# Weight splits and block 0's transposes as steps of each engine's order, with the orders laid out anew, in a two-stage MLP kernel on one core

## The reference

```python
# attention part: a causal depthwise convolution with 7 softmaxed taps per token and head
w = softmax(weight_gen)                     # (2, 4096, 8 heads, 7 taps)
out = einsum('bshk,bskhg->bshg', w, windows of x)   # (2, 4096, 192)
x = out.reshape(8192, 192)
# first MLP
h = x @ w_in                                # 192 -> 2048
P = a[0] + a[1]*h + a[2]*h**2 + a[3]*h**3
Q = 1 + |b[0]|*|h| + |b[1]|*h**2
x = (P / (Q + 1e-6)) @ w_out                # 2048 -> 192
# second MLP
xn = x / rms(x) * rms_g
x = (silu(xn @ w_gate) * (xn @ w_val)) @ w2_out     # 192 -> 1536 -> 192
```

## Time and profile before

| | |
|---|---|
| median of 3 runs | 1444.26 us (1442.95 to 1446.41) |
| profiled execution | 1445.34 us |
| its span, first to last instruction | 1443.5 us |
| TensorE matmul busy | 1368.5 us, 95% |
| VectorE busy | 1247.1 us, 86% |
| ScalarE busy | 1071.0 us, 74% |
| GpSimd busy | 458.4 us, 32% |
| granted TensorE clock, mean | 0.983 |

### The profile page before, as it was taken

How to read it: one execution, slowest core, us unless ns; L and a number is a source line. 1 busy time by engine, 2 the same in 40 slices (tenths; PEclk the granted TensorE clock), 3 DMA queues, 4 the chain that set the end, 5 groups by cost and what they waited for, 6 DMA issues and landing times.

```text
span 1443.5 us, 20421 instructions
## 1 busy us (share of the span) xinstructions
PE 1368.5 (95%) x7040; PEld 1221.0 (85%) x7040; DVE 1247.1 (86%) x1524; ACT 1071.0 (74%) x1387; POOL 458.4 (32%) x283
## 2 busy tenths in 40 slices
PE   2676999999999999999999999999999999999999
PEld 2465898888898888889898888989888898998988
DVE  6999998989889898988989899898989989888621
ACT  4676877878787787888778788877878787777521
POOL 2935240434324143432414343241434314200000
PEclk9788999999999999999999999999999999999999
DMA  8200001000000100000010000001000000000000
GB/s 232 82 0 31 1 2 41 1 32 11 30 11 0 41 0 30 11 30 11 0 41 0 30 11 30 11 0 41 0 30 11 30 12 0 12 0 1 12 12 11
DMA packets 12514, 32.30 MB, mean 22 GB/s; under 512 B 1604, under 2 KB 7234, under 8 KB 12480
## 3 DMA queue, kind: packets, MB, share of 16 engines
q1 hardware_dynamic: 11744, 31.61, 6.8%
q10 hardware_dynamic: 736, 0.23, 0.1%
HBM read 25.55 MB, written 6.29 MB: 22 GB/s over the span
## 4 chain that ended last, share of the span: by engine, by line
PE 76%; DVE 11%; ACT 7%; issue 4%; DMA 2%; SPq 0%; ACTq 0%; POOL 0%; DVEq 0%; POOLq 0%
PE dn L681 32%; PE bank L672 9%; PE bank L673 8%; PE bank L674 8%; PE bank L675 8%; PE bank L676 8%; DVE den L607 4%; ACT seed L484 2%; PE bank L688 2%; DVE num L599 2%; DVE num L596 1%; DVE num L612 1%; DVE num L618 1%; ACT L484 1%; DMA glu<-in_moe_w_val_dram 1%
## 5 line engine op out<-in xcount | busy, mean ns | idle before, releaser
L681 PE MATMUL dn<-dn_w,num 128*128 128x192 f32 x2048 | 378.8, 329 | 17.1 <-DVE num L618 9.9
L681 PEld LDWEIGHTS dn<-dn_w,num 128*128 128x128 f32 x2048 | 343.5, 192 | 24.3 <-DVE num L618 8.6
L469 ACT ACTIVATE den<-bank,coef 128x512 f32<-128x512 f32 x256 | 175.5, 686 | 175.8 <-PE bank L676 164.6
L681 PE MATMUL dn<-dn_w,glu 128*128 128x192 f32 x1536 | 280.8, 327 | 5.3 <-DVE glu L643 5.3
L681 PEld LDWEIGHTS dn<-dn_w,glu 128*128 128x128 f32 x1536 | 254.3, 190 | 12.9 <-DVE glu L643 8.9
L596 DVE TENSOR_TENSOR num<-num,bank 128x512 f32<-128x512 f32 x256 | 173.9, 679 | 70.1 <-ACT num L471 68.1
L612 DVE SCALAR_TENSOR_TENSOR num<-num,coef,seed 128x1024 f32<-128x1024 f32 x128 | 183.5, 1435 | 40.8 <-ACT seed L490 40.3
L471 ACT ACTIVATE num<-bank,coef 128x512 f32<-128x512 f32 x256 | 199.5, 779 | 0.0
L618 DVE SCALAR_TENSOR_TENSOR num<-den,num 128x1024 f32<-128x1024 f32 x128 | 193.1, 1510 | 0.0
L597 DVE SCALAR_TENSOR_TENSOR den<-den,coef,bank 128x512 f32<-128x512 f32 x256 | 188.9, 738 | 0.0
L599 DVE SCALAR_TENSOR_TENSOR num<-num,coef,bank 128x512 f32<-128x512 f32 x256 | 188.9, 738 | 0.0
(11 more groups left out here) (86 smaller groups left out, 1983.4 us busy)
## 6 DMA issues: line engine op xcount, KB each, us to landing
x_in<-in_x_dram SPq DMA_DIRECT2D x14, 960.0 KB
out_dram<-y_out SPq DMA_DIRECT2D x16, 384.0 KB, 2.3
...
dn_w<-in_moe_w_out_dram SPq DMA_DIRECT2D x1, 1152.0 KB, 10.6
...
seed<-in_moe_w_gate_dram SPq DMA_DIRECT2D x1, 768.0 KB, 10.0
```

The source lines that it names most:

```text
L681: done = pe.matmul(banks[:, j // 2, j % 2 * D:(j % 2 + 1) * D], acts[:, j * P:(j + 1) * P], w, start=first and j % 2 == 0, stop=last, skip ...
```

## The change

- All eight pieces become steps: `high` n on ScalarE, `low` n on VectorE (0 to 3) and on GpSimd (4 to 7), each done once, in the turn that its lag names. GpSimd no longer waits for VectorE's four splits ahead of its own.
- Block 0's flips, x_high and x_low become steps like those of the other blocks; xpose, x_high and x_low leave FROM_BLOCK.
- On GpSimd, block 1's mul and add stand between low 4, 5, 6 and 7.
- All four orders, the banks and BEFORE are new. The turn now begins at another step (lags are smaller by one behind it on TensorE), and inside the turn steps have changed places.

```diff
 ACT_PROGRAM = program("""
-... silu 0 3, silu 1 3, abs 7 2, silu 2 3, silu 3 3, exp 0 0,
-linear 0 1, root 3 2, square 6 2, silu 4 3, linear 1 1, piece 6 0, square 7 2, ...
-abs 5 1, xn_high 1 2, linear 12 1, linear 13 1, root 2 1, linear 14 1, x_high 0 0, linear 15 1, y 0 3,
+high 0 0, linear 13 2, high 4 1, linear 14 2, linear 15 2, square 5 2, x_high 0 1, x_high 1 1, abs 6 2,
+abs 7 2, silu 0 3, silu 1 3, silu 2 3, high 5 1, exp 0 0, root 3 2, linear 0 1, y 0 4, square 6 2,
+linear 1 1, silu 3 3, silu 4 3, linear 2 1, linear 3 1, square 7 2, abs 0 1, silu 5 3, linear 4 1, abs 1 1,
 ...
-ONCE = ("piece",)
+ONCE = ("high", "low")
 FROM_BLOCK = {"peak": 2, "less": 2, "exp": 2, "inverse": 2, "norm": 2,
-              "mul": 1, "add": 1, "xpose": 1, "x_high": 1, "x_low": 1}
+              "mul": 1, "add": 1}
 ...
             pool.wait_ge(conv0_ready, 1)
             pool.memset(x_in[:, 0:(HALO - SLOTS) * D], 0.0).then_inc(halo0, 1)
-            pool.wait_ge(wlo0, BY_DVE)
-            for n in range(BY_DVE, len(PIECES)):
-                piece_low(0, n)
 ...
             exponentials(0, 0)
-            for n in range(5):
-                piece_high(0, n)
-            x_high(0, 0)
-            x_high(0, 1)
-            piece_high(0, 5)
-            act.wait_ge(coefs, 2)
 
             def linear(blk, c):
                 h = bank[UP1_BANK[c]][:, :]
+                if isinstance(blk, int) and (blk, c) == (0, 0):
+                    act.wait_ge(coefs, 2)
 ...
             for k in range(K):
                 first_taps(k)
-            for n in range(2):
-                piece_low(n)
 ...
             dve.wait_ge(coefs, 2)
-            x_low(0, 0)
-            x_low(0, 1)
-            for n in range(2, BY_DVE):
-                piece_low(n)
 ...
             def up1(blk, c):
                 if c == 0:
+                    if isinstance(blk, int) and blk == 0:
+                        pe.wait_ge(wlo0, 2)
                     wait(pe, x_ready, blk * 2 + 2)
 ...
             pe.wait_ge(consts, 3)
-            transposes(0, 0)
-            transposes(0, 1)
-            pe.wait_ge(wlo0, 2)
```

More of the change, by code:

```diff
@@ L32 @@
 PE_PROGRAM = program("""
[L33 to L37, removed]
@@ L38 @@
-down1 1 1, xnx 0 2, down2 9 3, down1 2 1, xnx 1 2, down1 3 1, up1 12 1, up1 13 1, up1 14 1, up1 15 1,
-down1 4 1, down2 10 3, xpose 0 0, down1 5 1, down2 11 3, down1 6 1, xpose 1 0, down1 7 1, gate 0 2, gate 1 2,
-value 0 2, gate 2 2, gate 3 2,
+down1 6 1, xpose 0 0, xpose 1 0, down1 7 1, gate 0 2, gate 1 2, gate 2 2, value 0 2, value 1 2, gate 3 2,
+up1 0 0, gate 4 2, up1 1 0, down1 8 1, down2 0 2, down1 9 1, down2 1 2, down1 10 1, up1 2 0, value 2 2,
+up1 3 0, value 3 2, down2 2 2, gate 5 2, up1 4 0, value 4 2, value 5 2, up1 5 0, down1 11 1, down2 3 2,
@@ L41 @@
+down1 12 1, gate 6 2, up1 6 0, up1 7 0, down1 13 1, down2 4 2, down1 14 1, down2 5 2, down1 15 1, gate 7 2,
+gate 8 2, value 6 2, value 7 2, up1 8 0, up1 9 0, up1 10 0, down1 0 0, down2 6 2, gate 9 2, value 8 2,
+gate 10 2, value 9 2, up1 11 0, gate 11 2, value 10 2, value 11 2, down1 1 0, down2 7 2, xnx 0 1, down1 2 0,
+down2 8 2, down1 3 0, down2 9 2, xnx 1 1, up1 12 0, up1 13 0, up1 14 0, up1 15 0, down1 4 0, down2 10 2,
+down1 5 0, down2 11 2,
 """)
 ACT_PROGRAM = program("""
-square 4 2, x_high 1 1, square 5 2, abs 6 2, silu 0 3, silu 1 3, abs 7 2, silu 2 3, silu 3 3, exp 0 0,
@@ new lines @@
+abs 7 2, silu 0 3, silu 1 3, silu 2 3, high 5 1, exp 0 0, root 3 2, linear 0 1, y 0 4, square 6 2,
+linear 1 1, silu 3 3, silu 4 3, linear 2 1, linear 3 1, square 7 2, abs 0 1, silu 5 3, linear 4 1, abs 1 1,
+linear 5 1, root 0 1, square 0 1, linear 6 1, square 1 1, high 6 1, abs 2 1, silu 6 3, linear 7 1, ss 0 2,
+silu 7 3, silu 8 3, linear 8 1, linear 9 1, high 1 0, high 7 1, abs 3 1, linear 10 1, silu 9 3, silu 10 3,
+root 1 1, linear 11 1, high 2 0, abs 4 1, square 2 1, square 3 1, silu 11 3, abs 5 1, xn_high 0 2, root 2 1,
@@ L50 @@
+xn_high 1 2, square 4 1, linear 12 1, high 3 0,
 """)
 DVE_PROGRAM = program("""
[L53 to L56, removed]
@@ L57 @@
-glu 6 3, qy 1 1, newton 0 1, glu 7 3, newton 1 1, xn 0 2, horner 8 1, horner 9 1, horner 10 1, glu 8 3,
-glu 9 3, py 2 1, qy 2 1, glu 10 3, horner 11 1, newton 2 1, qy 3 1, glu 11 3,
+newton 3 3, horner 12 3, horner 13 3, horner 14 3, horner 15 3, peak 0 1, x_low 0 2, x_low 1 2, qy 4 3,
+low 3 2, py 4 3, py 5 3, glu 0 4, newton 4 3, glu 1 4, qy 5 3, low 2 1, inverse 0 1, newton 5 3, qy 6 3,
+py 6 3, horner 0 2, horner 1 2, glu 2 4, horner 2 2, horner 3 2, newton 6 3, glu 3 4, qy 7 3, glu 4 4,
+py 7 3, horner 4 2, horner 5 2, glu 5 4, newton 7 3, py 0 2, qy 0 2, py 1 2, qy 1 2, newton 0 2, horner 6 2,
@@ L59 @@
+horner 7 2, glu 6 4, newton 1 2, glu 7 4, xn 0 3, horner 8 2, horner 9 2, horner 10 2, glu 8 4, low 0 0,
+glu 9 4, horner 11 2, glu 10 4, py 2 2, py 3 2, qy 2 2, qy 3 2, newton 2 2, glu 11 4, xn_low 0 3, xn_low 1 3,
+low 1 0,
 """)
 POOL_PROGRAM = program("""
-add 6 1, less 0 0, norm 0 0, mul 0 0, mul 1 0, mul 2 0, add 1 0, mul 3 0, add 2 0, mul 4 0, rms 0 2, add 3 0,
-mul 5 0, add 4 0, mul 6 0, add 5 0,
-""")
-UP1_BANK = (1, 3, 0, 2, 1, 3, 1, 3, 0, 1, 3, 2, 1, 2, 3, 0)
-GATE_BANK = (3, 0, 2, 3, 2, 0, 2, 1, 3, 2, 0, 3)
@@ L68 @@
-VALUE_BANK = (1, 0, 1, 3, 2, 0, 0, 2, 1, 2, 0, 1)
-XPOSE_BANK = (1, 2)
-XNX_BANK = (3, 0)
-BEFORE = {
-    ("value", 1): ("gate", 1, 1), ("up1", 0): ("value", 0, 1), ("gate", 4): ("gate", 2, 1),
[3 rows of a table removed]
[L78 to L88, removed]
+less 0 0, norm 0 0, mul 0 0, low 5 1, mul 1 0, mul 2 0, add 1 0, rms 0 2, mul 3 0, add 2 0, mul 4 0, low 6 1,
@@ L430, in _ @@
             run_iterations(pool, POOL_PROGRAM, {"mul": tap_product, "add": tap_add, "rms": rms_inverse,
-                                                "less": peak_taken_off, "norm": normalised_taps}, LAST)
+                                                "less": peak_taken_off, "norm": normalised_taps,
+                                                "low": piece_low}, LAST)
         @block.scalar
@@ L540, in softmax_inverse, with piece_low @@
                 dve.reciprocal(total, guarded).then_inc(sm_inverse, 1)
-            def piece_low(n):
+            def piece_low(_, n):
                 dve.wait_ge(whi, n + 1)
@@ L648, in _ @@
                 "xn": normalised, "xn_low": xn_low, "glu": glu_product,
-                "peak": softmax_peak, "inverse": softmax_inverse}, LAST)
+                "peak": softmax_peak, "inverse": softmax_inverse, "low": piece_low}, LAST)
         @block.tensor
```

23 lines of the change are left out of this document (22 added, 1 removed), and 3 rows, old and new, of the table BEFORE.

## The result

The changed kernel takes **1483.28 us** in the median (1483.17 to 1483.79, 4 runs), the one before 1444.2 in the runs beside it (1442.95 to 1446.41): a ratio of 1.027, 95% interval 1.0252 to 1.0287. Slower by 39 us; 1481 was forecast. The profiled execution took 1483.79 us, its span 1482.0, 38.5 more than the span before.

The account below looks back on a forecast made before the run. VectorE was taken to bound the kernel before 160.9 us, TensorE after. Span 1443.5 + 12 (beginning) + 25.5 (turns) = 1481.0, so a time of 1481 us; the forecast's own range 1463 to 1495, the wider one 1451 to 1500.

Parts of the forecast that it names:

- Value 2 waits for horner 0: Loop turns: TensorE's value 2 starts at 16.3 us instead of 14.45, its bank held until horner 0; stall 1.85 us.
- less the 0.45 us: Twelve turns: the old wait of glu's second-layer chunk for VectorE's product falls away, 0.45 us each, 5.4 in all.
- The floor of y: Each turn: down2 0, at 8.1 us, waits for y, which ends at 9.0; 0.9 us lost even without GpSimd.
- 0, give or take 1: The end, gates of blocks 14 and 15: same steps, each reader early enough, so no change within 1 us.
- Block 0's turn: First unrolled turn: table loaded only after qy 5, horner 0 done at 18.1 us, a stall of 3.7 us.
- The beginning: Up to gate 0 of block 0, 160.9 us before: +12 us, bounds +9 and +14.
- The gain at linear 0: Block 0's linear 0 right behind split 5 frees up to 4.9 us; taken as lost as low 2 waits for low 4.
- The way to block 1's x_low: Beginning: GpSimd's splits among convolution products and two more holes move block 1's first x_low from 89.34 to about 97.4, +8.
- the rms part: Block 1, within its +4 us: GpSimd's rms stands three steps earlier, keeping nine instead of six convolution steps behind it.
- turns nearly free: Rival: beginning dear, turns cost only y's floor, +5, or nothing; 1455 us, chance 0.20.
- dearer turns: Rival: qy 6 misses its 0.6 us margin, so the loop's turns cost 3.7 too; +18, 1500 us, chance 0.09.
- Faster: Rival: GpSimd doesn't get between, horner 0 starts 3.65 us sooner, turns take 83.8 instead of 84.6; 1431 us, chance 0.12.

Follow-up runs that it names:

- experiment 2: Changed kernel with VectorE's horner 0 moved ahead of qy 6 and py 6: 1467.18 us, ratio 1.0149.
- experiment 4: Changed kernel with most of GpSimd's convolution left out from block 3 on (the output changes): 1469.39 us, ratio 1.0155.
- experiment 3: Changed kernel with both moves, y ahead of x_high 0 and horner 0 ahead of qy 6: 1447.83 us, ratio 1.0014.
- experiment 1: Changed kernel with ScalarE's y moved ahead of x_high 0: 1473.64 us, ratio 1.0191.
- horner_first: The kernel of experiment 2: changed kernel with horner 0 ahead of qy 6 and py 6, 1467.18 us.
- Old_start: The kernel of experiment 8: changed kernel with GpSimd's four splits together ahead of block 1's convolution, 1477.32 us.
- experiment 7: Changed kernel in which GpSimd's low 4 waits again for VectorE's four splits: 1480.85 us, ratio 1.0246.
- experiment 8: Changed kernel with experiment 7's wait, GpSimd's splits together ahead of block 1's convolution, ScalarE's pieces 6 and 7 behind linears 1 and 3: 1477.32 us, ratio 1.0227.
- y_early: The kernel of experiment 1: changed kernel with ScalarE's y ahead of x_high 0, 1473.64 us.
- low4_late: The kernel of experiment 7: changed kernel with low 4 waiting again for VectorE's four splits, 1480.85 us.
- experiment 5: Changed kernel with a one-element activation loading root's table ahead of root 3's waits in the unrolled turns: 1472.22 us, ratio 1.0182.

## Why the prediction was right

**Value 2 waits for horner 0.** Right in the loop, step by step, to 0.1 us; experiments 2 and 4 show both its halves (the place, and GpSimd's convolution beside it). Mis-sized is what it costs. Forecast were 1.4 us net a turn, measured 0.94. The stall is 16.17 − 14.45 = 1.72 (14.45 is when value 2 starts in experiment 3, as forecast), against 1.85. The larger error is the base: "less the 0.45 us" took the recorded wait of the earlier trace rows for all that a turn had to give. Without any wait the new turn is 83.63, 0.95 under the old one of 84.58; 83.63 + 1.72 gives 85.35 of the 85.52 measured. Of the 0.95, 0.76 goes with the wait, since the old turn without it took 83.81 (the first in the earlier trace rows); the rest is left to TensorE's new order. Other recorded waits, too, stood for some 0.3 us more than themselves: y's 0.73 in experiment 2 for 1.01 (84.64 against 83.63), horner 0's 1.55 in experiment 1 for 1.86 (85.49 against 83.63). Ten turns: 4.6 us too much.

**The floor of y.** The prediction priced it at 0.9 and put it under horner 0's lateness. It is 1.0 by experiments 2 and 3 (84.64 against 83.63), and right in the loop. The step that failed is the one outside it: there the root and so y are 1.3 us later, and down2 0 waits 2.1 us. The text gave y no time of its own in these turns. In block 12's turn that changed little: qy 6 asked 11.25 us after value 0, the add got in ahead of py 6 as forecast, and horner 0, done at 17.8 (forecast 18.1), was still the last. In block 1's turn it was done at 17.9, but TensorE, held up by y and then by its clock, came to value 2 only at 18.46, so the +3.1 there is near the forecast for a reason that is in part another. In block 13's turn, where no convolution lifts horner 0 above it, y is the bound (+3.8 instead of 1.3), and in block 14's, "0, give or take 1", down2 0 comes sooner for want of the next block's up1, and waits 3.1 us: +5.1. Experiment 1 gives both back to the end (83.38, 54.17).

**The clock behind a stall.** No term for it. In the changed kernel the same wait of 2.1 us at down2 0 was followed by a lower clock in block 1's turn but not in block 12's. The windows, two of each:

```profile
269.00:275.00 6.00, 3.94 (x19) 3.54 (x18) 1.69 (x2) 6.00 (x7) 5.78 (x5) 0.89 0.16 66
275.00:281.00 6.00, 6.00 (x31) 5.83 (x30) 6.00 (x6) 2.50 (x4) 2.55 (x1) 0.83 0.00 1
...
1212.00:1218.00 6.00, 3.94 (x23) 3.56 (x23) 1.69 (x2) 5.98 (x8) 5.87 (x5) 1.00 0.16 66
1218.00:1224.00 6.00, 5.10 (x29) 4.45 (x28) 6.00 (x7) 3.70 (x5) 2.29 (x1) 1.00 0.00 0
```

Its price is seen where nothing else differs: in horner_first, blocks 12 and 13 have the same wait for y, and value 2 started 16.79 and 18.46 us after value 0. That is 1.67 us, with these windows:

```profile
1196.00:1206.00 10.00, 7.94 (x46) 7.42 (x45) 7.30 (x8) 9.37 (x11) 8.72 (x5) 1.00 0.10 39
1282.00:1292.00 10.00, 7.94 (x36) 7.41 (x35) 6.62 (x9) 9.36 (x11) 0.00 (x0) 0.83 0.11 41
```

Old_start has the changed kernel's orders in block 13's turn and the same wait of 2.1 us; there the clock stayed at 1.00, and the turn took 85.11 us instead of 86.78, again 1.67 less. Old_start's window first, then the changed kernel's:

```profile
1292.50:1302.50 10.00, 7.94 (x47) 7.44 (x46) 4.97 (x8) 8.68 (x11) 0.00 (x0) 1.00 0.11 41
1299.00:1309.00 10.00, 7.94 (x37) 7.53 (x37) 5.04 (x7) 8.53 (x11) 0.00 (x0) 0.83 0.11 41
```

So block 13's +3.8 is y's stall of 2.1 us and 1.7 for the clock. Block 14's +5.1 is a stall of 3.1, and 2.0 that are left for the clock and what a recorded wait leaves out; no run separates these. The turn of the loop in the windows after the change, with its two short waits, stayed at 1.00.

**Block 0's turn.** +4.4 for +3.7, but not by the forecast path: 1.4 us of waiting for silu 3, which no term names, 1.1 for horner 0 (value 2 at 17.38, not 18.1), and a clock of 0.67 from 190 to 195 us. That the sum is near is luck.

**The beginning.** +12 forecast, +10.0 measured, near the lower bound. The gain at linear 0 was eaten at the door as forecast (experiment 7 takes the door away: 3.6 us at horner 0), by the neighbour of the instruction that was named. The way to block 1's x_low: +6.9 for +8, and experiment 8 gives all of it back. Block 1: +3.1 for +4. Horner 0's place is the main part of it, but its size is uncertain. Where its place is the changed kernel's, the way from x_low to gate 0 took 74.6 us, and 73.7 in y_early and low4_late; with horner 0 moved it took 72.6 (experiment 2) and 71.6 (experiment 3, whose orders are the same up to there, as the first y comes later). So two executions of the same orders differ by 1 us, and the move gives 1 to 3. The earlier table load of experiment 5 gives 1 to 2 as well (72.6), and the rms part stays open.

**Of the rivals,** "turns nearly free" falls with the waits above, "dearer turns" with qy 6 asking at 9.92, 0.7 us before the door opens. The sum of "turns nearly free" doesn't follow from its own terms: with +5 for the turns it is 1461, and 1455 holds only for turns that cost nothing. "Faster" needed VectorE not to be kept waiting; experiment 3 shows what it had right, a laid-out turn of 83.63.

**The sum.** 38.5 for 37.5 is nearer than its parts. The beginning, the loop and block 12's turn were forecast 7 us too dear, block 0's turn and the two at the end 8 us too cheap. The mechanism of the beginning and of the loop is shown; that the total came within 2.3 us of 1481 is luck.
